# A chained attention and two-layer mixture-of-experts kernel: weight splits moved, idle TensorE time filled with products, weight transfers issued from the tile ends

## The reference

```python
def _attn_ref(r, k, v, w, u):                      # (2, 8, 768, 48)
    for t in range(S):
        cur = np.einsum('bhd,bhe->bhde', u[None] * kt, vt)
        y[:, :, t] = np.einsum('bhd,bhde->bhe', rt, state + cur)
        state = w[None, :, :, None] * state + np.einsum('bhd,bhe->bhde', kt, vt)

def _moe_ref(x, modality_id, w_gate, modality_bias, w1, w2):
    logits = x @ w_gate + modality_bias[modality_id]
    e_idx = np.argmax(logits, axis=1)
    gate_w = softmax(logits)[np.arange(N), e_idx]
    for e in range(E):
        h = np.maximum(x[mask] @ w1[e], 0.0)       # mask: e_idx == e
        out[mask] = gate_w[mask, None] * (h @ w2[e])

def _moe2_ref(x, w_gate, w1, w2, capacity):        # capacity 384
    # as above without the bias; a token beyond the expert's capacity gives 0
```

## Time and profile before

| | us |
|---|---|
| median of 3 runs (403.66 to 403.96) | 403.79 |
| the profiled execution | 403.24 |
| its span, from the first to the last instruction | 401.1 |
| PE busy | 357.1 (89%) |
| DVE busy | 214.6 (53%) |
| POOL busy | 183.6 (46%) |
| ACT busy | 138.8 (35%) |

### The profile page before, as it was taken

The page is one execution under the profiler, slowest core; times in us unless marked ns, Lnnn a source line. Parts: engine busy times, 40 slices in busy tenths (PEclk is TensorE's granted clock), DMA queues, the critical chain, the costliest instruction groups (busy, mean ns, idle before and its releaser), DMA issues.

```text
span 401.1 us, 10500 instructions
## 1 busy us (share of the span) xinstructions
PE 357.1 (89%) x3162; PEld 346.9 (86%) x3163; DVE 214.6 (53%) x555; ACT 138.8 (35%) x229; POOL 183.6 (46%) x303
## 2 busy tenths in 40 slices
PE   0699899955999999999999999459999999999990
PEld 0589789945899999999999999349999999999990
DVE  5378567689198855555555558492412454334310
ACT  2266445525145522222222233103324555245220
POOL 6797799913155633333333336141732444444311
PEclk9999999985699999999999999868999999999996
DMA  6999976124799311111111241118629999393000
GB/s 127 174 322 287 240 164 138 39 86 150 241 409 402 142 40 40 40 40 40 40 40 40 60 176 25 32 42 319 216 75 360 324 315 334 122 342 131 30 26 16
DMA packets 68234, 62.03 MB, mean 155 GB/s; under 512 B 45493, under 2 KB 61028, under 8 KB 68080
## 3 DMA queue, kind: packets, MB, share of 16 engines
q1 hardware_dynamic: 60800, 48.85, 38.6%
q0 software_dynamic: 3744, 10.23, 7.8%
q10 hardware_dynamic: 3664, 2.62, 2.1%
HBM read 52.85 MB, written 10.14 MB: 157 GB/s over the span
## 4 chain that ended last, share of the span: by engine, by line
PE 69%; POOL 12%; issue 7%; DVE 6%; DMA 2%; ACT 1%; POOLq 0%; ACTq 0%; DVEq 0%; SPq 0%
PE p_h L1199 37%; PE p_o L1221 28%; POOL sc L554 5%; POOL prod L541 3%; PE p_xt L1177 3%; POOL r_sc L536 2%; POOL prod L543 1%; DMA w_col<-in_w 1%; DMA xg<-x_rows,src_idx 1%; DVE row_oh L370 1%; DVE pinv L782 0%; DVE w_lo L831 0%; DVE til_id L919 0%; DVE st L817 0%; DVE pw L779 0%
## 5 line engine op out<-in xcount | busy, mean ns | idle before, releaser
L1199 PE MATMUL p_h<-xT,w_sb 128*128 128x128 f32 x1296 | 153.3, 280 | 1.4 <-ACT xT L656 1.4
L1199 PEld LDWEIGHTS p_h<-xT,w_sb 128*128 128x128 f32 x1296 | 152.5, 196 | 2.0 <-issue 2.0
L984 DVE SCALAR_TENSOR_TENSOR h_lo<-p_h,h_hi 128x512 fp32r<-128x512 f32 x54 | 37.3, 692 | 84.7 <-ACT h_hi L743 83.6
L1001 DVE CUSTOM_DVE_ANT_0 lg_prod<-y_row,wg_all 128x384 f32<-128x384 f32 x112 | 55.7, 553 | 41.2 <-ACT y_row L753 41.1
L1221 PE MATMUL p_o<-w_hi,h_hi 128*128 x216 | 74.9, 347 | 0.0
L1221 PE MATMUL p_o<-w_hi,h_lo 128*128 x216 | 72.7, 336 | 0.0
L1221 PE MATMUL p_o<-w_lo,h_hi 128*128 x216 | 72.6, 336 | 0.0
L743 ACT ACTIVATE h_hi<-p_h 128x512 fp32r<-128x512 f32 x54 | 32.3, 598 | 114.7 <-PE p_h L1199 108.9
L566 POOL TENSOR_TENSOR dst_mark<-zeros 128x1 f32<-128x1 f32 x54 | 14.4, 266 | 103.8 <-DVE y_row L1001 67.1
L831 DVE TENSOR_TENSOR w_lo<-w_raw,w_hi 128x1024 fp32r<-128x1024 f32 x36 | 43.7, 1266 | 7.5 <-ACT w_hi L656 6.1
L566 POOL TENSOR_TENSOR src_mark<-zeros 128x1 f32<-128x1 f32 x54 | 19.0, 351 | 55.5 <-PE p_xt L1177 34.6
(11 more groups left out here) (189 smaller groups left out, 400.2 us busy)
## 6 DMA issues: line engine op xcount, KB each, us to landing
w_raw<-in_moe_w SPq DMA_DIRECT2D x12, 1536.0 KB
w_sb<-in_moe_w SPq DMA_DIRECT2D x12, 1536.0 KB
k_raw<-in_k SPq DMA_DIRECT2D x12, 192.0 KB, 3.7
r_raw<-in_r SPq DMA_DIRECT2D x12, 192.0 KB, 3.7
v_raw<-in_v SPq DMA_DIRECT2D x12, 192.0 KB, 3.9
x_rows<-x_rows SPq DMA_DIRECT2D x12, 192.0 KB, 2.3
out<-zeros ACTq DMA_DIRECT2D x1, 2304.0 KB, 10.3
wg_nat<-in_moe_w_gate SPq DMA_DIRECT2D x1, 1536.0 KB, 6.4
```

Source lines behind the costliest of these rows:

```text
L984: stt(h_lo[:, at, :], p_h[n][:, :, :], 0.0, h_hi[:, at, :].bitcast(F32), ALU.max, ALU.subtract).then_inc(h_ready[layer], 1)
L1001: last = nv.tensor_tensor_reduce(out=lg_prod[:, n, :], in0=y_row[par][:, 0:DM], in1=wg2_all[:, e, :], op0=ALU.mult, op1=ALU.add, scale=1.0 ...
L1199: last = mm(p_h[half][:, f, :], w1_sb[place][:, c, col:col + P], xT[:, c, :], start=(c == 0), stop=(c == DC - 1))
```

## The change

- Attention: the two `split_low` inside units 2 and 3 and the one before the logits are gone; all three stand after layer 0's `route`, ahead of the tiles.
- The two transfers of zeros leave ACT's queue. SP issues those for `x2` after `wg2_nat`, and those of the output after the weights of layer 0's experts. SP's first load waits also for `zeros_set`.
- PE: `keep_clock` takes a bank and a count and stands in nine kinds of place: 50 products before the power transposes, 12 after the first `turn_kr`, 48 before layer 0's `route`; in both layers 36 after the ranks, 34 after `place_ids`, 18 after the wait for the plan, 4 after the first `turn_x`; 8 and 14 around the last tile's logits.
- The plan: the tables for SP are gone. `ends` signals `ends_known`; ACT copies the eight ends to `plan_ends`; SP loads all eight into registers at once and decides from them. For the first expert after the one that is loaded, SP issues W1 first and both without a wait in layer 0. In layer 1 the wait for the W2 buffer is one that is long met.
- ACT: the copy to `wg2_all` is cut into four pieces of two experts each: two after `turn_x` in tile 0 of layer 0, ahead of the W2 split, two after `y_row`. `row_logits` waits for all four.

```diff
@@ constants
-    WARM = 36
+    WARM_SETUP, WARM_TURN, WARM_LAST, WARM_RANK, WARM_PLACE, WARM_PLAN, WARM_FIRST = 50, 12, 48, 36, 34, 18, 4
+    WARM_Y, WARM_LOGITS = 8, 14
+    WG_PIECES = 4
@@ SP
             sp.wait_ge(ones_set, 1)
+            sp.wait_ge(zeros_set, 1)
...
-            def expert(layer, planned, e, read_layer, read_e):
-
-                num = sp.value_load(plan_num[planned][0:1, bass.ds(e, 1)], min_val=1, max_val=2 * E)
-                split = sp.value_load(plan_split[planned][0:1, bass.ds(e, 1)], min_val=1, max_val=2 * NPC * E)
+            def expert(planned, read_layer, read_e):
+
+                n = sp.snap(num, min_val=1, max_val=2 * E)
+                free = sp.snap(older_end, min_val=0, max_val=NSLOT)
                 for place in range(2):
-                    with sp.If((num & 1) > 0 if place else (num & 1) < 1):
-                        sp.wait_ge(w2_ready, split)
-                        expert_w2(place, read_layer, read_e)
-                        free = sp.value_load(plan_free[planned][0:1, bass.ds(e, 1)], min_val=0, max_val=2 * NSLOT)
+                    with sp.If((n & 1) > 0 if place else (n & 1) < 1):
+                        with sp.If(free < 1):
+
+                            expert_w1(place, read_layer, read_e)
+                        with sp.If(n > 1):
+                            sp.wait_ge(w2_ready, NPC * (n - 1))
+                            expert_w2(place, read_layer, read_e)
+                        with sp.If(n < 2):
+
+                            expert_w2(place, read_layer, read_e)
                         with sp.If(free > 0):
-                            sp.wait_ge(h_made[planned], free)
+                            sp.wait_ge(h_made[planned], 2 * free)
                             expert_w1(place, read_layer, read_e)
...
+                sp.wait_ge(ends_sent, layer + 1)
+                sp.load(end_regs, plan_ends[layer][0:1, :])
+                end = [sp.snap(r, min_val=0, max_val=NSLOT) for r in end_regs]
...
+                for e in range(1, E):
+                    with sp.If(end[e] > end[e - 1]):
+                        expert(layer, layer, e)
...
             sp.dma_start(wg2_nat[:, :, :], wg2.partition_broadcast(P)).then_inc(wg2_spread, 16)
+            sp.dma_start(x2[:, DM:XW].rearrange("(c p) e -> p c e", p=P),
+                         zeros[:, 0:E].unsqueeze(1).broadcast_to([P, NT, E])).then_inc(x2_zeroed, 16)
+            sp.reg_mov(num, 1)
+            experts(0)
+            sp.dma_start(out.rearrange("(c p) d -> p c d", p=P),
+                         zeros[:, :].unsqueeze(1).broadcast_to([P, NT, DM])).then_inc(out_zeroed, 16)
+            expert(0, 1, 0)
+
             sp.wait_ge(plan_known, 1)
-            experts(0)
-            expert(1, 0, E, 1, 0)
@@ ACT
-                if isinstance(n, int) and n == RING - 1:
-
-                    act.dma_start(out.rearrange("(c p) d -> p c d", p=P),
-                                  zeros[:, :].unsqueeze(1).broadcast_to([P, NT, DM])).then_inc(out_zeroed, 16)
-                    act.dma_start(x2[:, DM:XW].rearrange("(c p) e -> p c e", p=P),
-                                  zeros[:, 0:E].unsqueeze(1).broadcast_to([P, NT, E])).then_inc(x2_zeroed, 16)
...
+                act.wait_ge(ends_known, layer + 1)
+                copy(plan_ends[layer][0:1, :], ends[0:1, 1:E + 1]).then_inc(ends_sent, 1)
...
+            def router_weights(pieces):
+
+                act.wait_ge(wg2_spread, 16)
+                for n in pieces:
+                    at = slice(n * E // WG_PIECES, (n + 1) * E // WG_PIECES)
+                    copy(wg2_all[:, at, :], wg2_nat[:, :, at].rearrange("p d e -> p e d")).then_inc(wg2_turned, 1)
...
                 turn_x(layer, j + 1)
+                if layer == 0 and first:
+                    router_weights(range(WG_PIECES // 2))
...
                     .then_inc(y_scaled[layer], 1)
+                if layer == 0 and first:
+                    router_weights(range(WG_PIECES // 2, WG_PIECES))
 
             exponentials(0)
-            act.wait_ge(wg2_spread, 16)
-            copy(wg2_all[:, :, :], wg2_nat[:, :, :].rearrange("p d e -> p e d")).then_inc(wg2_turned, 1)
@@ DVE
-                if isinstance(n, int) and n > 1:
-
-                    split_low(0, 0, [n - 2])
...
-                    dve.wait_ge(wg2_turned, 1)
+                    dve.wait_ge(wg2_turned, WG_PIECES)
...
-            split_low(0, 0, range(RING - 2, NPC))
-
...
             route(0, lg)
+            split_low(0, 0)
@@ PE
-            pe.wait_ge(consts, 1)
+            def keep_clock(at, count):
+
+                for n in range(count):
+                    mm(at[:, 0:P], ones_b[:, :], before_b[:, :], start=(n == 0), stop=(n == count - 1))
+
+            pe.wait_ge(consts, 2)
+            keep_clock(p_x[:, 0, :], WARM_SETUP)
...
                 last.then_inc(ranked, 1)
+                keep_clock(p_o, WARM_RANK)
                 place_ids(layer)
...
+                keep_clock(p_o, WARM_PLACE)
+                pe.wait_ge(plan_known, layer + 1)
+                keep_clock(p_o, WARM_PLAN)
...
+            keep_clock(p_o, WARM_LAST)
             route(0)
-            keep_clock()
```

More of the change, by code:

```diff
@@ L457, in _ @@
                 store(n, n % B, n // B)
[L459 to L470 removed]
+            end_regs = [sp.alloc_register(f"end{e}") for e in range(E)]
@@ L899, in route @@
                 ch.do(nv.reduce_sum(tiles[:, :], over[:, :, :], axis=AX.X))
-                ch.do(nv.tensor_tensor_scan(ends[:, 1:E + 1], ones_e[:, :], tiles[:, :], 0.0, ALU.mult, ALU.add))
+                nv.tensor_tensor_scan(ends[:, 1:E + 1], ones_e[:, :], tiles[:, :], 0.0, ALU.mult, ALU.add).then_inc(ends_known, 1)
+                dve.wait_ge(ends_known, layer + 1)
                 dve.wait_ge(ranked, layer + 1)
@@ L1120, in unit @@
                 turn_kr(n, b)
+                if isinstance(n, int) and n == 0:
+                    keep_clock(p_x[:, 0, :], WARM_TURN)
                 if not (isinstance(n, int) and n < 2):
@@ L1185, in router_turn_y @@
                 last.then_inc(y_turned, 1)
+                keep_clock(p_o, WARM_Y)
             def tile(layer, j, par, what):
@@ L1223, in tile, with first_x @@
                 last.then_inc(y2_made[layer], 1)
+            keep_clock(p_o, WARM_LAST)
             route(0)
-            keep_clock()
             pe.wait_ge(router_in, 16 * N_ROUTER)
-            last = all_tiles(pe, 0, tile, lambda: turn_x(0, 0, 0), code_next)
+            def first_x(layer):
+                turn_x(layer, 0, 0)
+                keep_clock(p_o, WARM_FIRST)
+            last = all_tiles(pe, 0, tile, lambda: first_x(0), code_next)
             for par in range(2):
```

40 lines of the change are left out of this document (12 added, 28 removed).

## The result

The changed kernel is slower: 409.3 us median of 5 runs (406.64 to 410.86) against 403.79 before, a ratio of 1.0132 (95% interval 1.0082 to 1.0183). The prediction was 408.6. I read both.

A forecast was written before the change was run, and what follows sets the result against it. PE was taken to bound the expert tiles, PE and POOL attention, a planning-and-gather chain the hand-overs. Terms summing to +4.8 us on the profiled 403.24 gave 408.0, shifted to a median of 408.6 us; range 398.3 to 412.3.

The forecast's parts named there:

- 1, 2: to unit 11's scores: Attention: start wait against warming products +0.1 us; splits and zeros leaving the units -2.4 us.
- 3: last third of the split: Before the logits: the last third of the W2 split goes from the front of them, -1.0 us.
- 4: products before the one-hots: Before layer 0's one-hots: 48 warming products cost +0.2 us, which faster counting gives back; nothing net.
- 5: first hand-over: Layer 0, attention to expert tiles: early weights delay the gather, first p_h again near 8.15 us; +1.6 us.
- 6: pieces, tile 1: Layer 0, tile 1: four router-weight pieces on ACT delay h_lo, so PE waits for p_o; +3.6 us.
- 7: clock behind the hole: After PE's wait in tile 1: the clock may fall, price 0 to 2.8 us; taken as +1.3 us.
- 8: second hand-over: Into layer 1's tiles: gather late behind weights +1.2 us, slower first p_h +0.4 us; +1.6 us.
- Start: Kernel start: SP's added wait for zeros costs at most 0.4 us, 50 products worth about as much; taken as +0.1 us.
- Gathers: Both hand-overs: the first gather, running under expert weights, loses 2.5 us, between bounds of 0 and 3.4 us.
- Their early sending buys nothing.: Layer 0's expert weights: no p_h ever waited for weights, so sending them early gains nothing.
- B: Rival, both hand-overs: gathers not held up, landing below about 4 us; 398.9 us in all, chance 0.17.
- C: Rival, tile 1: gathers late but the pieces quick, below 0.8 us, or fitting; 404.6 us, chance 0.15.

The follow-up runs named there:

- e12: The changed kernel run and profiled again, but for a masked register: 410.28 us, ratio 1.016 to before.
- e10: The kernel before with the zeros moved to SyncE's queue and the three W2 splits after layer 0's routing: 400.06 us, ratio 0.9895.
- e4: The changed kernel with the warming products as before, 36 after place_ids and none elsewhere: 411.29 us, ratio 1.0153.
- e5: The kernel of e3 with the second expert's W2 issued ahead of its W1: 396.7 us, ratio 0.9825.
- e11: The kernel of e5 with the router weights' load issued earlier and the gather wait directly ahead of the first W2: 394.6 us, ratio 0.9777.
- e1: The changed kernel with the router weights turned by one copy ahead of the tiles, not four pieces: 405.18 us, ratio 1.0008.
- e2: The changed kernel with SP sending no weights before the layer's first gather has landed; the pieces stay: 407.96 us, ratio 1.0083.
- e3: The changed kernel with the edits of e1 and e2 together: 403.23 us, ratio 0.9953.
- e6: The kernel of e5 with W2 sent once the ends are known and W1 and the rest after the first gather: 402.91 us, ratio 0.996.
- e8: The kernel of e5 with the warming products as before, 36 after place_ids only: 400.76 us, ratio 0.9934.
- e7: The kernel before with only the three W2 splits moved behind layer 0's routing: 403.38 us, ratio 0.9989.
- e9: The kernel before with only the zeros moved from ScalarE's queue to SyncE's: 401.92 us, ratio 0.9953.

## Why the prediction came out

The direction, the forecast's mechanisms and the median (408.6 against 409.3) were right; several sizes were not, and their misses partly cancel. By its own terms, with the two profiles of the changed kernel (after / e12):

| term | predicted | measured |
|---|---|---|
| 1, 2: to unit 11's scores | -2.3 | -2.9 / -2.9 |
| 3: last third of the split | -1.0 | -1.4 / -1.4 |
| 4: products before the one-hots | 0 | 0 / 0 |
| 5: first hand-over | +1.6 | +1.2 / +0.8 |
| 6: pieces, tile 1 | +3.6 | +3.6 / +3.6 (e12's +6.0 less the row below) |
| 7: clock behind the hole | +1.3 | 0 / +2.4 |
| 8: second hand-over | +1.6 | +1.6 / +2.0 |
| not in the sum | 0 | +1.3 / +1.8 |
| sum | +4.8 | +3.5 / +6.2 |

**Start.** I gave the added wait 0.4 us and the products as much. Runs price them apart: without products, unit 0's scores stand at 16.47 in e10 (without the wait) and 16.96 in e4 (with it), so the wait costs 0.5; in after, with both, they stand at 15.94, so the products brought 1.0 there and 1.7 by unit 2. I had judged that PE idled too long before 16.5 us. But this is a gain by execution: of the eight profiled executions with the products at the start, four have the scores of unit 11 at 75.8 to 75.9 us (after, e5, e11, e12) and four at 77.1 to 78.7 (e1, e2, e3, e6), where e10, e4 and e8, without them, have 77.15, 77.62 and 78.06. The mean of the eight is 76.9, that is -1.9 against before; my -2.3 lies closer to it than the -2.9 of the two profiles in the table. What decides between the two groups was not tried. The slice with its digit 6 shows that the clock was not kept throughout; it need not be, to gain.

**Attention.** That PE is what is late from unit 2 on was exact (48.24 us). But the step credited the splits and took the zeros as included. e7 shows that the splits alone would have given -1.4 for the last third and +1.5 inside, e9 that the zeros alone give -1.2 inside. The attribution was wrong though the sum of both edits was right.

**Gathers.** The price was 3.5 (3.1) and 3.4 us, above the 2.5 that I took and at the upper bound from the earlier trace rows. My reason for less, that a gather has its reads delayed only once, failed. From the one-hots to the first p_h it took 2.7 us (e12: 2.0) more than before in layer 0 and 2.3 (2.0) more in layer 1, where I had 1.6 and 1.2. The first p_h went the other way (6.6 and 6.5 us, in e12 6.8 and 6.9, where I had 8.15 and about 7.6). The products around the plan may have kept part of the clock; e1, with the same products and a first p_h of 7.80 and 7.46 us, speaks against a sure effect. In both layers two misses cancelled, to 0.8 us or less: that the terms came out was luck. The light reading of the Trainium skill's "DMA: Bandwidth & Descriptors" (Arbitration), by which the gather would wait little, is refuted for this traffic: 3.2 to 4.0 us with no expert weights ahead of it in e2, e3, e5 and e11, 5.2 to 6.1 behind 1.5 MB, 6.2 to 6.9 behind 3 MB.

**"Their early sending buys nothing."** Right against before, though I had seen only half of it. I looked at whether a p_h waits for W1; the one who waits is ScalarE's split, for W2, and the change put W2 second. Had the weights been sent late in that order, a hole of 3.5 us would have come (e3). I listed "W1 first" in the change and gave it no price.

**Pieces.** The term was exact to 0.1 us, from a queue run by hand with the row of 5.77 us: the pieces took 1.6 us each where I had 1.45, which ScalarE made up for by coming to them some tenths sooner. The step was confirmed by e1. What the Trainium skill's "SBUF — State Buffer" (SBUF cachelines) says of reads that leave a 16-byte line each time agrees with this pace: 6.4 us for 3072 columns, where the split's same number takes 2.96.

**Clock behind the hole.** A mean was taken for something that happens or not. The two profiles show both ends, 0 and 2.4 of my 0 to 2.8.

**Signs.** The first weights went 3.5 us ahead of the gather (4 forecast), the gather landed after 6.9 (5.5 to 6.8 forecast), the first p_h took 6.6 (8 forecast), p_o of tile 1 waited 3.04 (3), unit 11's scores came at 75.92 (76.4 to 77). The slice of tile 1 printed no clock below 9 in after's profile; in e12's it did.

**Rivals.** B (gathers not held up) would have needed a landing below 4 us: seen only where the weights wait. What B says of the first p_h then came true: 5.6 us in both layers in e2, e3 and e11, where it had 5.36. C needed pieces below 0.8 us: they took 1.6.

## What to carry to other kernels

Before a large transfer is sent earlier, ask who else uses the DMA engines in the freed time, and what small transfer is on the path there: a gather of 0.2 MB lost 3.4 us behind 3 MB which nobody was waiting for. When several transfers share a queue, order them by who needs them first (here the split of W2, not the product with W1): that exchange was worth some 5 us, as much as taking the four pieces out of tile 0. And two causes in a row in one queue hide each other: removing the first alone may gain nothing (e7), so read the wait that stands behind it before crediting the edit.

## What the runs showed beyond that

**Two weights sent one behind the other landed in order of issue.** Of two weights of 1.5 MB issued 0.5 to 0.7 us apart, the first landed 6.4 to 7.4 us after its issue and the second 11.6 to 12.4, whichever of W1 and W2 it was (e2, e3, e5, e11).

**Tiles have two periods.** In the steady tiles a period is either 9.85 or 9.92 us, all of it in p_o, while p_h takes 5.36 us in both. Two lines of the chain of after, layer 0 and layer 1, both at a granted clock of 1.00:

```profile
151.09 4.16 PE p_o L1237 x24
...
301.35 4.24 PE p_o L1237 x24
```

One layer keeps one period from about its third tile on. Before had the shorter one in both layers, e12 the longer one in both, after and e1 the shorter one first, e5 the longer one first; the same kernel had it otherwise in its two profiles. The three kernels built on before (e7, e9, e10) and e11 had the shorter one in both layers. It is worth up to 1.8 us an execution and explains part of the spread between runs. What decides it was not tried, and stays open.
